# Three tiles of the leading expert worked out ahead of the full routing, instead of four

## The chip, the cores and the metric

The kernel runs on one core of a Trainium2 chip. The metric is the device time of one execution in microseconds (us). Engines are named as in the profile: PE is TensorE, ACT ScalarE, DVE VectorE, POOL GpSimd, SP SyncE.

## What is computed

Three layers in a row, on 4 sequences of 576 tokens with 512 channels (8 heads of 64):

```
q_s = softmax(q, axis=-1);  k_s = softmax(k, axis=2)
attn = q_s @ (k_s^T @ v)                                   # per head; 4 x 576 x 512
h = relu(x^T @ w_tok1) @ w_tok2;  u = x + h^T              # mixing over the tokens
x1 = u + relu(u @ w_ch1) @ w_ch2                           # 512 -> 1536 -> 512 channels
logits = x1 @ w_gate                                       # 8 experts
e[s] = argmax(logits[s]) where sigmoid(x1[s] @ w_local) < 0.5 or s == 0, else e[s-1]
out[s] = softmax(logits[s])[e[s]] * (relu(x1[s] @ w1[e]) @ w2[e])      # 512 -> 1024 -> 512
```

## The kernel before, in words

Every engine runs its own hand-ordered list of instructions; semaphores tie them together. What one engine waits for holds up all that stands behind it on that engine.

**Part one** works through the batches b = 0 to 3. The channel layer of a batch is 32 "chunks": per half of the tokens 12 chunks of the hidden layer (`hid`, 12 matmuls each) and 4 of its output (`y`, 36 matmuls each), numbered by `idx` 0 to 31. Products are kept nearly exact by splitting each operand into a rounded part (name with `_h`) and a rest (`_l`): ACT writes `hid_h`, DVE `hid_l`, for each chunk. PE may start chunk idx only when the outputs of chunk idx-2 are out (`chan_done`). Between the chunks of batch b stand the attention steps of batch b+1 for two groups of heads. The table `AT` (L304) says behind which chunk each step stands, on every engine that has a share in it, and the same table serves all three batches that have a next one. The steps spoken of below, all for group 0:

- `kmax` and `kmax2` (DVE, L1164): the maximum of the keys. `kmax` is one operation of 512 columns; `kmax2` is two of 256 columns into the tile shown as `lgp`. PE's step `mT` (`kmax_turn`, L517), behind chunk 5, transposes what `kmax2` leaves.
- `qT01` and `qT23` (PE, L547): ten transposes of the normalized queries. The first two need the first half of POOL's scaling (`pool_scale`, L1802, operation L1794), the next three the second half.

The weights of the channel layer are split once, at the start. ACT rounds them, and the rests `wc_l` of the 12 pieces of `w_ch2` are made by DVE for the even pieces (`split_second`) and by POOL for the odd ones (L1821), beside the first chunks.

**Part two** is the expert layer. Tokens of one expert are gathered into tiles of 128 rows. For a tile t PE does `hidden` (two halves of 12 matmuls, L783), transposes it (`h_turn`, L795), and does `output` (two halves of 12 matmuls, L808); `x_turn` (L725) transposes the gathered rows. DVE makes the rests `xgT_l` (`xgT_out`, before hidden half 0) and `hT_l` (`hT_out`, before output) and scales the result (`yo_out`). POOL gathers the rows of a tile and scatters its result with indirect DMAs.

Which token goes where is known only when the logits of all batches are. So a first routing of batches 0 to 2 (`route_early`) picks the expert with most tokens there, and its first `EARLY` tiles are run by straight-line code. Beside them DVE works out the full routing: `held_by_lanes`, `tiles_of_experts`, `rows_of_lanes`, `tiles_of_lanes`, `probabilities`, `values_of_lanes`, `row_lanes`. PE turns that into row numbers (`rows_of_tiles`, L826, 18 matmuls), DVE stores them (`ids_out`), POOL gathers tile number `EARLY`, and from there a loop over a table of tiles runs (`Fori`, L894) until all tiles are done. If the leading expert had fewer full tiles than `EARLY`, the missing ones would be run empty (`unfilled`). SP loads an expert's weights in 8 units of 512 KB; for the second expert it starts once the gathers of tiles `EARLY` and `EARLY + 1` have landed (L501 to L503), and ACT and DVE split the units inside the tiles.

## Time and profile before

| | us |
|---|---|
| median of 3 runs (728.61 to 729.15) | 728.89 |
| the profiled execution, its own time | 728.89 |
| its span in the profile | 726.8 |
| PE busy | 715.9 |
| DVE busy | 304.6 |
| ACT busy | 234.5 |
| POOL busy | 137.5 |

The 2.09 us between the span and the execution's own time lie outside what the profiler records. Times in the rows are microseconds from the start of the span. Part one runs until about 455, the early tiles until about 512, the loop of tiles from there.

### The profile page before, as it was taken

To read this page: it belongs to the slowest core of one execution; us is meant where nothing else is said; L and a number is where in the kernel's file an instruction comes from. 1 tells how busy PE (TensorE), PEld (TensorE's weight loads), DVE (VectorE), ACT (ScalarE), POOL (GpSimd) and SP (SyncE) were. 2 spreads that over 40 slices of the span, in tenths; PEclk is the share of its full clock that TensorE was granted. 3 is DMA by queue.
4 is the path that set the end of the run, shared out by engine and by line. 5 is a ranking of instruction groups with operands and counts; after the bars stand their busy time and mean duration, and the time that the engine had idled before them with its cause. 6 is when DMAs were issued, how large, how long until landed. Compare 5 with 4: busy or idle time off the path is not lost.

```text
span 726.8 us, 14345 instructions
## 1 busy us (share of the span) xinstructions
PE 715.9 (99%) x5016; PEld 650.9 (90%) x5017; DVE 304.6 (42%) x641; ACT 234.5 (32%) x452; POOL 137.5 (19%) x166
## 2 busy tenths in 40 slices
PE   7999999999999999999999999999999999999997
PEld 7799999999999999999999999788888888888885
DVE  5765332235332235332224822685445552221631
ACT  2773142023142023142021034321445542222621
POOL 5574020002020002020000016022221322121311
PEclk9999999999999999999999999999999999999999
DMA  9952131012131012100010340113744561010000
GB/s 224 376 108 67 33 99 33 1 35 67 33 99 33 1 35 67 33 33 1 1 38 2 116 163 16 54 44 125 289 159 139 180 238 58 23 52 29 34 22 12
DMA packets 71997, 57.65 MB, mean 79 GB/s; under 512 B 54892, under 2 KB 57228, under 8 KB 71952
## 3 DMA queue, kind: packets, MB, share of 16 engines
q1 hardware_dynamic: 68432, 47.58, 21.9%
q0 software_dynamic: 3520, 9.44, 3.9%
q8 instruction: 32, 0.52, 0.3%
q14 instruction: 13, 0.11, 0.0%
HBM read 48.79 MB, written 10.31 MB: 81 GB/s over the span
## 4 chain that ended last, share of the span: by engine, by line
PE 96%; DVE 2%; ACT 1%; issue 1%; POOL 0%; POOLq 0%; DVEq 0%
PE bank L640 42%; PE bank L783 16%; PE bank L808 15%; PE bank L572 5%; PE bank L603 3%; PE bank L795 2%; PE bank L595 2%; PE bank L671 2%; PE bank L725 1%; PE bank L515 1%; PE bank L543 1%; PE bank L560 1%; PE bank L582 1%; PE bank L648 1%; PE bank L529 0%
## 5 line engine op out<-in xcount | busy, mean ns | idle before, releaser
L640 PE MATMUL bank<-u_h,wc_h 128*128 128x288 f32 x384 | 117.2, 305 | 0.1
L640 PE MATMUL bank<-hid_h,wc_h 128*128 128x288 f32 x384 | 115.0, 300 | 0.0
L640 PE MATMUL bank<-hid_l,wc_h 128*128 128x288 f32 x384 | 113.2, 295 | 0.0
L640 PE MATMUL bank<-u_h,wc_l 128*128 128x288 f32 x384 | 113.1, 295 | 0.0
L640 PE MATMUL bank<-u_l,wc_h 128*128 128x288 f32 x384 | 113.1, 294 | 0.0
L640 PE MATMUL bank<-hid_h,wc_l 128*128 128x288 f32 x384 | 113.0, 294 | 0.0
L783 PE MATMUL bank<-wslots,xgT_h 128*128 (+1 forms) x344 | 110.6, 402 | 0.0
L808 PE MATMUL bank<-wslots,hT_h 128*128 (+1 forms) x336 | 104.2, 391 | 0.1
L1485 DVE SCALAR_TENSOR_TENSOR hid_l<-bank,hid_h 128x288 fp32r<-128x288 f32 x96 | 43.1, 454 | 108.7 <-ACT hid_h L989 108.2
L989 ACT ACTIVATE hid_h<-bank 128x288 fp32r<-128x288 f32 x96 | 39.3, 409 | 113.5 <-PE bank L640 113.1
L808 PEld LDWEIGHTS bank<-wslots,hT_h 128*128 128x128 f32 x336 | 62.6, 188 | 13.6 <-DVE hT_l L1691 0.7
L640 PEld LDWEIGHTS bank<-u_h,wc_h 128*128 128x128 f32 x384 | 72.1, 188 | 1.8 <-DVE hid_l L1485 1.0
L640 PEld LDWEIGHTS bank<-hid_h,wc_l 128*128 128x128 f32 x384 | 72.3, 188 | 0.0
L640 PEld LDWEIGHTS bank<-u_l,wc_h 128*128 128x128 f32 x384 | 72.2, 188 | 0.1
L640 PEld LDWEIGHTS bank<-hid_l,wc_h 128*128 128x128 f32 x384 | 72.2, 188 | 0.1
L640 PEld LDWEIGHTS bank<-hid_h,wc_h 128*128 128x128 f32 x384 | 72.0, 188 | 0.1
L640 PEld LDWEIGHTS bank<-u_h,wc_l 128*128 128x128 f32 x384 | 72.0, 188 | 0.0
L783 PEld LDWEIGHTS bank<-wslots,xgT_h 128*128 128x128 f32 x344 | 61.4, 189 | 11.3
L783 PE MATMUL bank<-wslots,xgT_l 128*128 (+1 forms) x172 | 67.8, 394 | 0.0
L808 PE MATMUL bank<-wslots,hT_l 128*128 (+1 forms) x168 | 65.6, 390 | 0.0
L1492 DVE TENSOR_TENSOR x1T<-bank,u_h 128x288 f32<-128x288 f32 x32 | 14.6, 457 | 115.7 <-PE bank L640 115.7
L1868 POOL DMA_INDIRECT out_dram<-yo,id_out x21 | 22.8, 1084 | 172.1 <-DVE yo L1702 172.1
(270 smaller groups left out, 1056.6 us busy)
## 6 DMA issues: line engine op xcount, KB each, us to landing
w1raw<-in_moe_w_dram SPq DMA_DIRECT2D x20, 512.0 KB, 5.3
w2raw<-in_moe_w_dram SPq DMA_DIRECT2D x20, 512.0 KB, 4.8
wc_raw<-in_moe_w_ch_dram SPq DMA_DIRECT2D x8, 768.0 KB, 10.3
vb<-in_v_dram SPq DMA_DIRECT2D x32, 128.0 KB, 3.2
x_rows<-x1n SPq DMA_DIRECT2D x16, 256.0 KB
kb<-in_k_dram SPq DMA_DIRECT2D x24, 128.0 KB, 2.9
qb<-in_q_dram SPq DMA_DIRECT2D x24, 128.0 KB, 2.9
qraw<-in_q_dram SPq DMA_DIRECT2D x2, 512.0 KB, 4.7
```

The costliest lines, as they stand in the source:

```text
L572: last = pe.matmul(mix_bank(n, g)[:, c * TOK:(c + 1) * TOK], queries(n)[:, i, c * P:(c + 1) * P], wt1[:, i, :], start=(i == 0), stop=(i == ...
L595: pe.matmul(bank[4 + j % 2][:, 0:HS], kvd[:, c // CG, c % CG, :], qT[:, c // CG, c % CG, part], start=True, stop=False)
L603: last = pe.matmul(bank[4 + j % 2][:, 0:HS], h1T[a][:, m, c * P:(c + 1) * P], wt2[x][:, m, part], start=False, stop=(m == KT - 1 and (a, x ...
L640: last = pe.matmul(to, lhsT, rhs, start=(m == 0), stop=(m == len(mms) - 1))
L671: last = pe.transpose(bank[7][0:size, c * P:(c + 1) * P], x1T[:, c, at:at + size], ident[:, :])
L783: last = pe.matmul(bank[half][:, :], xgT[a][:, c, :], w1s[x][:, bass.ds(n & 1, 1), c, half * 512:(half + 1) * 512].rearrange("p a n -> p ( ...
L795: last = pe.transpose(bank[2 + half][:, c * P:(c + 1) * P], hs[:, f * P:(f + 1) * P], ident[:, :])
L808: last = pe.matmul(bank[5][:, :], hT[a][:, f, :], w2s[x][:, bass.ds(n & 1, 1), f, :].rearrange("p a n -> p (a n)"), start=(f == 0 and (a, ...
L989: act.activation(hid[0][:, i, :], bank[idx % 2][:, 0:HS], ACT.Relu).then_inc(hid_hi, 1)
L1485: dve.scalar_tensor_tensor(out=hid[1][:, i, :], in0=psum, scalar=0.0, in1=hid[0][:, i, :], op0=ALU.max, op1=ALU.subtract).then_inc(chan_do ...
L1492: dve.tensor_tensor(x1T[:, i, :], psum, u[0][:, i, part], ALU.add).then_inc(y_sum, 1)
L1868: pool.indirect_dma_start(out=out.rearrange("b s d -> (b s) d"), out_offset=bass.IndirectOffsetOnAxis(ap=id_out[:, 0:1], axis=0), in_=yo[: ...
```

## The change

`EARLY` goes from 4 to 3. The straight-line code of tile 3 goes away on all engines and the loops begin at tile 3. PE's `rows_of_tiles` moves from behind the second `h_turn` of tile 2 to ahead of its first. On DVE `tiles_of_experts` and `rows_of_lanes` become one function, `slots_of_lanes`, and the pieces of the routing and the work for the tiles are interleaved in another order. On POOL the gathers of tiles 3 and 4 now stand ahead of the scatter of tile 1. In part one DVE makes the rests of pieces 0 to 4 of `w_ch2` and POOL those of 5 to 11, and three entries of the table `AT` change.

```diff
-    EARLY = 4
+    EARLY = 3
...
-        BY_VECTOR = (0, 2, 4, 6, 8, 10)
-        BY_POOL = (1, 3, 5, 7, 9, 11)
+        BY_VECTOR = 5
...
-            ("kmax", 0): 3, ("kmax2", 0): 3, ("mT", 0): 5, ("ksub", 0): 6, ("ksub2", 0): 6, ("kexp", 0): 6,
+            ("kmax", 0): 3, ("kmax2", 0): 4, ("mT", 0): 5, ("ksub", 0): 6, ("ksub2", 0): 6, ("kexp", 0): 6,
...
-            ("qrec2", 0): 7, ("kv", 0): 9, ("qT01", 0): 11, ("qT23", 0): 12, ("mix", 0): 12, ("h1", 0): 13,
+            ("qrec2", 0): 7, ("kv", 0): 9, ("qT01", 0): 10, ("qT23", 0): 11, ("mix", 0): 12, ("h1", 0): 13,
...
+            rows_of_tiles()
             h_turn(2, 0, True)
             hidden(2, 0, 1, True)
-            x_turn(3)
-            output(2, 0, 0, True)
+            output(2, 0, 0, True, FIRST)
             h_turn(2, 1, True)
-            rows_of_tiles()
...
-                if j in (3, 5, 7):
-                    split_second(j - 3)
+                if j >= 2 * KD - BY_VECTOR:
+                    split_second(j - (2 * KD - BY_VECTOR))
             for idx in range(HEAD):
                 chunk_out(0, idx)
-                split_second(2 * KD - 2 + 2 * idx)
...
+            probabilities(P, 2)
+            yo_out(0, False)
+
             hT_out(1, 0)
-            yo_out(0, False)
-
-            tiles_of_experts()
+            slots_of_lanes()
             xgT_out(2)
-            rows_of_lanes()
             tiles_of_lanes()
             hT_out(1, 1)
-            probabilities(P, 2)
             values_of_lanes()
+            row_lanes(P, rowhot, rows_hot)
             yo_out(1, True)
...
-            for c in BY_POOL:
+            for c in range(BY_VECTOR, KC):
...
             gather(2, EP * J)
             scatter(0, False)
-            pool.wait_ge(xgT_ready, 3)
-            gather(3, EP * J)
-            scatter(1, True)
...
             gather(EARLY, rows_in=xg3, id_of=id_in3, landed=x3_in)
-            pool.wait_ge(xgT_ready, EARLY)
+            pool.wait_ge(xgT_ready, 3)
             gather(EARLY + 1)
+            scatter(1, True)
```

Three places of the order of instructions. DVE beside chunks 3 and 4 of the first batch, before:

```order
L1485 SCALAR_TENSOR_TENSOR hid_l<-bank,hid_h 128x288
L1172 TENSOR_TENSOR kmax<-kb 128x512
L1175 TENSOR_TENSOR lgp<-kmax 128x256
L1178 TENSOR_TENSOR lgp<-lgp,kb 64x256
L1485 SCALAR_TENSOR_TENSOR hid_l<-bank,hid_h 128x288
L1214 TENSOR_REDUCE qmax<-qb 128x8
```

and with the change:

```order
L1470 SCALAR_TENSOR_TENSOR hid_l<-bank,hid_h 128x288
L1157 TENSOR_TENSOR kmax<-kb 128x512
L1470 SCALAR_TENSOR_TENSOR hid_l<-bank,hid_h 128x288
L1160 TENSOR_TENSOR lgp<-kmax 128x256
L1163 TENSOR_TENSOR lgp<-lgp,kb 64x256
L1199 TENSOR_REDUCE qmax<-qb 128x8
```

The two `lgp` operations (`kmax2`) now stand behind the `hid_l` of chunk 4, and so behind the end of that chunk on PE.

PE at the first ten transposes of the queries, before (the chunk behind them is the first `y` chunk):

```order
L640 MATMUL bank<-u_h,wc_h 128x288
L640 MATMUL bank<-u_l,wc_h 128x288
L640 MATMUL bank<-u_h,wc_l 128x288
L560 MATMUL bank<-ident,qb 128x128 x5
L640 MATMUL bank<-hid_h,wc_h 128x288
L640 MATMUL bank<-hid_l,wc_h 128x288
```

and with the change (behind them comes chunk 11 of the hidden layer):

```order
L639 MATMUL bank<-u_h,wc_h 128x288
L639 MATMUL bank<-u_l,wc_h 128x288
L639 MATMUL bank<-u_h,wc_l 128x288
L559 MATMUL bank<-ident,qb 128x128 x5
L639 MATMUL bank<-u_h,wc_h 128x288
L639 MATMUL bank<-u_l,wc_h 128x288
```

The five transposes of `qT01` moved one chunk of 12 matmuls ahead.

DVE in early tile 1, from the end of `held_by_lanes` (`held`, `own`) on, before:

```order
L1579 CAST held<-upto 128x8
L1344 TENSOR_TENSOR own<-chosen,code 128x144
L1691 TENSOR_TENSOR hT_l<-bank,hT_h 128x512
L1702 TENSOR_SCALAR yo<-bank,prob_t 128x512
L1584 TENSOR_TENSOR gt<-bank,step 128x144
```

and with the change (`den` to `prob_l` are `probabilities`):

```order
L1329 TENSOR_TENSOR own<-chosen,code 128x144
L1334 TENSOR_REDUCE den<-expl 128x18
L1335 TENSOR_TENSOR top<-expl,own 128x144
L1336 TENSOR_REDUCE prob<-top 128x18
L1337 TENSOR_SCALAR den<-den 128x18
L1338 RECIPROCAL den<-den 128x18
L1339 TENSOR_TENSOR prob<-prob,den 128x18
L1340 CAST prob_h<-prob 128x18
L1341 TENSOR_TENSOR prob_l<-prob,prob_h 128x18
L1684 TENSOR_SCALAR yo<-bank,prob_t 128x512
L1673 TENSOR_TENSOR hT_l<-bank,hT_h 128x512
L1568 TENSOR_TENSOR gt<-bank,step 128x144
```

The first `hT_l` of tile 1 moved behind the eight operations of `probabilities` and behind `yo` of tile 0; the operations of `slots_of_lanes` from `gt` on follow it, and the `xgT_l` of tile 2 stands behind all of them.

## Rows read from the trace of the kernel before

**Rows 1.** The page's busy times, and the longest of PE's four waits.

```profile
PE 715.9 (99%) x5016; PEld 650.9 (90%) x5017; DVE 304.6 (42%) x641; ACT 234.5 (32%) x452; POOL 137.5 (19%) x166
...
PE bank L515 <- POOL kvd L1783: 3.6, 1, 3.6
```

**Rows 2.** Timeline, batch 0: start, duration, engine, line, tiles, count; POOL, DVE, PE.

```profile
51.16 1.54 POOL L1823 TENSOR_TENSOR wc_l<-wc_raw,wc_h 128x512 fp32r<-128x512 f32 x1 [0.16 <-ACT wc_h L1044]
...
52.03 1.23 DVE L1172 TENSOR_TENSOR kmax<-kb 128x512 f32<-128x512 f32 x1
...
54.22 0.44 PE L522 MATMUL bank<-ident,lgp 128*128 128x128 f32 x2
```

**Rows 3.** Timeline, batch 1, the same step; DVE, ACT, PE.

```profile
161.43 0.68 DVE L1172 TENSOR_TENSOR kmax<-kb 128x512 f32<-128x512 f32 x1
162.14 0.42 DVE L1175 TENSOR_TENSOR lgp<-kmax 128x256 f32<-128x256 f32 x1
162.60 0.42 DVE L1178 TENSOR_TENSOR lgp<-lgp,kb 64x256 f32<-64x256 f32 x1
...
162.19 0.41 ACT L989 ACTIVATE hid_h<-bank 128x288 fp32r<-128x288 f32 x1 [1.17 <-PE bank L640]
...
163.57 0.38 PE L522 MATMUL bank<-ident,lgp 128*128 128x128 f32 x2
```

**Rows 4.** Timeline, batch 1, POOL's scaling; PE at chunk 10 and at `qT01`.

```profile
171.75 2.47 POOL L1794 TENSOR_TENSOR qb<-qb,qrec 128x512 f32<-128x512 f32 x2 [4.33 <-DVE qrec L1225]
...
172.03 0.40 PE L640 MATMUL bank<-u_h,wc_h 128*128 128x288 f32 x1
...
175.30 0.71 PE L560 MATMUL bank<-ident,qb 128*128 128x128 f32 x5
```

**Rows 5.** Timeline, early tiles 1 and 2, DVE.

```profile
473.42 0.31 DVE L1344 TENSOR_TENSOR own<-chosen,code 128x144 f32<-128x144 int32 x1
...
474.65 0.74 DVE L1702 TENSOR_SCALAR yo<-bank,prob_t 128x512 f32<-128x512 f32 x1
476.13 0.31 DVE L1584 TENSOR_TENSOR gt<-bank,step 128x144 f32<-128x144 f32 x1 [0.74 <-PE bank L824]
...
477.53 0.69 DVE L1476 TENSOR_TENSOR xgT_l<-bank,xgT_h 128x512 fp32r<-128x512 f32 x1
478.14 0.15 DVE L1593 SCALAR_TENSOR_TENSOR before_p<-first_tile,bank 128x8 f32<-128x8 f32 x1
...
480.41 0.68 DVE L1605 TENSOR_TENSOR tilehot<-sloti,lane 128x504 f32<-128x504 int32 x1
...
481.74 0.29 DVE L1349 TENSOR_REDUCE den<-expl 128x18 f32<-128x144 f32 x1
...
483.64 0.68 DVE L1361 TENSOR_TENSOR val<-tilehot,token 128x504 fp32r<-128x504 f32 x1
```

**Rows 6.** Timeline, early tiles 1 and 2, PE.

```profile
476.34 0.71 PE L808 MATMUL bank<-wslots,hT_h 128*128 128x512 f32 x2
...
479.52 0.71 PE L783 MATMUL bank<-wslots,xgT_h 128*128 128x512 f32 x2
...
491.85 2.18 PE L830 MATMUL bank<-val,rowhot 128*128 128x84 f32 x18
```

**Rows 7.** Timeline, gather of tile 4; issue to landing of all 23 gathers.

```profile
495.55 1.10 POOL L1856 DMA_INDIRECT xg<-x_rows,id_in  x1 [0.86 <-POOL id_in L1853]
...
DMA to landing us min/median/max: 2.1/3.5/6.0
```

**Rows 8.** POOL's DMA queue from 478 to 486: packets, MB, share.

```profile
q0 software_dynamic: 152, 0.49, 20.1%
```

**Rows 9.** First weight units of the second expert (502 to 506); ACT's first split.

```profile
L417 SPq DMA_DIRECT2D w1raw<-in_moe_w_dram x4: 333/338/351, 502.8 to 504.8; - x4
...
DMA to landing us min/median/max: 3.8/6.7/7.8
...
513.74 2.01 ACT L983 ACTIVATE wslots<-w1raw 128x1024 f32 x2 [0.44 <-issue]
```

More of the change, by code:

```diff
@@ L243, in build @@
             yo = sb(part2, "yo", [P, D])
-            sb(part2, "end_of_rows", [P, 1104])
+            sb(part2, "end_of_rows", [P, 1120])
             xg3 = sb(part2, "xg3", [P, D])
@@ L614, in second_ready @@
             def second_ready(f):
-                if f in BY_VECTOR:
-                    pe.wait_ge(wc2_lo, BY_VECTOR.index(f) + 1)
+                if f < BY_VECTOR:
+                    pe.wait_ge(wc2_lo, f + 1)
                 else:
-                    pe.wait_ge(wc2_lo_pool, BY_POOL.index(f) + 1)
+                    pe.wait_ge(wc2_lo_pool, f - BY_VECTOR + 1)
             def chunk(b, idx, first=False):
@@ L860, in _ @@
             output(1, 0, 1, True)
+            rows_of_tiles()
             h_turn(2, 0, True)
             hidden(2, 0, 1, True)
-            x_turn(3)
-            output(2, 0, 0, True)
+            output(2, 0, 0, True, FIRST)
             h_turn(2, 1, True)
-            rows_of_tiles()
-            hidden(3, 0, 0, True)
-            output(2, 0, 1, True)
-            h_turn(3, 0, True)
-            hidden(3, 0, 1, True)
-            output(3, 0, 0, True, FIRST)
-            h_turn(3, 1, True)
             x_turn(EARLY)
-            output(3, 0, 0, True, SECOND)
-            output(3, 0, 1, True, FIRST)
+            output(2, 0, 0, True, SECOND)
+            output(2, 0, 1, True, FIRST)
             pe.wait_ge(routed, 2)
             hidden(EARLY, version_of(EARLY), 0, True)
-            output(3, 0, 1, True, SECOND)
+            output(2, 0, 1, True, SECOND)
             def tile(t, again):
@@ L1127, in _ @@
             hs_out(2, 1)
-            xgT_out(3)
             hT_out(2, 1)
-            hs_out(3, 0)
-            hT_out(3, 0)
-            hs_out(3, 1)
-            hT_out(3, 1)
             xgT_out(EARLY)
@@ L1579, in held_by_lanes, with slots_of_lanes @@
                 then(dve.tensor_copy(held[:, :], upto[SCANS % 2][:, PAD + J - 1, :]), expert_chosen)
-            def tiles_of_experts():
+            def slots_of_lanes():
                 dve.wait_ge(ranks_ready, 1)
@@ L1589, in tiles_of_experts @@
                 then(dve.tensor_reduce(first_tile[:, :], ntb[:, :, :], AX_X, ALU.add))
-            def rows_of_lanes():
                 then(dve.scalar_tensor_tensor(out=before_p[:, :], in0=first_tile[:, 0:E], scalar=float(P), in1=bank[7][:, E:2 * E], op0=ALU.mult, op1=ALU.add))
@@ L1715, in _ @@
             own_expert(P)
+            probabilities(P, 2)
+            yo_out(0, False)
             hT_out(1, 0)
-            yo_out(0, False)
-            tiles_of_experts()
+            slots_of_lanes()
             xgT_out(2)
-            rows_of_lanes()
             tiles_of_lanes()
             hT_out(1, 1)
-            probabilities(P, 2)
             values_of_lanes()
+            row_lanes(P, rowhot, rows_hot)
             yo_out(1, True)
+            ids_out()
             hT_out(2, 0)
-            row_lanes(P, rowhot, rows_hot)
-            xgT_out(3)
-            hT_out(2, 1)
-            ids_out()
             versions()
             tables()
-            yo_out(2, True)
-            hT_out(3, 0)
+            hT_out(2, 1)
+            xgT_out(EARLY)
             plan_loads()
-            hT_out(3, 1)
-            xgT_out(EARLY)
             word = next_weights(EARLY - 1)
@@ L1904, in _ @@
             gather(EARLY, rows_in=xg3, id_of=id_in3, landed=x3_in)
-            pool.wait_ge(xgT_ready, EARLY)
+            pool.wait_ge(xgT_ready, 3)
             gather(EARLY + 1)
+            scatter(1, True)
             scatter(2, True)
-            scatter(3, True)
             pool.wait_ge(routed, 2)
```

## Prediction

> **What bounds the kernel now.** I read the page's busy times first, then PE's waits, then the timeline of all engines at the three places that the change touches. The page says that PE is busy 99% of the span, and the longest of its four waits, 3.6 us, is at the very start [rows 1]; from 60 us to the last tile the list of its waits is empty. So PE sets the time, and its work stays what it was: the same chunks, and the same tiles as long as the fourth early tile is not an empty one. It isn't. In the 8 us in which tile 3 is gathered and tile 0 scattered, POOL's DMA queue moved 0.49 MB [rows 8], and two full tiles of 128 rows of 2 KB are 0.52 MB. A tile taken out of the straight code comes back as one more turn of the loop. A gain could come only from a wait of PE that goes, and there is none to go; what can change is that new waits appear. Since PE has no slack later, each one stays in the time to the end. The sum is made against the profiled execution: 726.8 us of span and 728.89 in all, which is also the median, so what is added to the span is added to 728.89.
>
> **Part one: kmax2 behind chunk 4, three times.** Uncontended case, batch 1 [rows 3]. Before, DVE ran kmax at 161.43 and the pair kmax2 right behind it, done at 162.60 + 0.42 = 163.02. PE came to its transposes at 163.57, so the margin was 0.55. Now the hid_l of chunk 4 stands between. It can't start before ACT's hid_h is out, 162.19 + 0.41 = 162.60, and takes until about 163.01 (0.38 from its start to DVE's next, as between 477.53 and 478.14 for a longer one). The pair then runs 0.46 + 0.42 (from 162.14 to 162.60, and the second's 0.42) and is done at 163.89. PE waits until about 163.95 with a handover of 0.06: 0.38 us. The same holds in batch 2. That is **+0.76** for two batches.
>
> Batch 0 is another case, since POOL is splitting weights there. Kmax took 1.23 us in batch 0 and 0.68 in batch 1 [rows 2, 3]. It started at 52.03 while a POOL split ran from 51.16 to 52.70, and it ended 0.55 late, so it had waited for nearly all of the 0.67 that the POOL operation still had to go. In these rows a DVE operation with two operands in SBUF waits until POOL's running one is through, and the other way round (POOL's splits take 1.30 alone and up to 1.73 beside one on DVE).
>
> The Trainium skill ("SBUF — State Buffer", section "SBUF: two separate sides") says the same of the port pair that the two share: an exclusive lock for the whole instruction, the loser fully blocked. This rule speaks against the change, and the rows agree; without it the step below would cost as little as its lower bound, with it the upper one.
>
> With the change POOL has seven pieces in one run instead of six with gaps. Piece 5 can't start before 45.9 us (ACT has it ready then); at 1.30 each, with 0.35 for the DVE split beside piece 5, POOL is at piece 9 from 51.5 to 52.8, at piece 10 from 53.3 (after kmax) to 54.6, and at piece 11 behind it. DVE comes to the pair at 53.67. Its first operation waits for piece 10 and is done at about 54.9; piece 11 has the port by then, until about 56.15; the second is done at 56.45. PE goes on with chunk 6 at 56.65, instead of 54.58 = 54.22 and the 0.36 that its transposes and the wait behind them took [rows 2]: **+2.07**. The low end: if neither operation meets POOL, the pair is done at 53.67 + 0.88 = 54.55, PE goes on at 54.75, and the step costs 0.17; with one meeting, 0.9. I take 2.07, since kmax's row shows the meeting and POOL's run leaves no gap for the second.
>
> **qT01 behind chunk 10, three times.** The transposes of its second tile need POOL's second scaling. In batch 1 that ended at 171.75 + 2.47 = 174.22 [rows 4]. PE began chunk 10 at 172.03 and reached qT01 at 175.30, after 24 matmuls, so a chunk is 1.64. Now qT01 comes at 173.67, the first tile's two transposes go until 173.83, and the rest waits until 174.29: 0.46. POOL's scaling hangs on chunk 6 through DVE, ACT and DVE again, so the delay from kmax2 moves both ends and does not cover this. Batches 0 and 2 repeat it within 0.02. **+1.4** for three. The bounds: none if this chain gains half a microsecond, 0.6 each if it loses a little.
>
> **The splits themselves** cost nothing beside this. DVE loses one of six; the last rest is ready at about 56.5 instead of 52.7, and PE reads the first of them in the first y chunk, ten microseconds later (near 67).
>
> **Part two: DVE's new order in early tile 1.** DVE had finished `own` at 473.42 + 0.31 = 473.73. Now the eight operations of the probabilities come next; they took 483.64 - 481.74 = 1.90 [rows 5]. Behind them yo of tile 0 (0.70 to the next) and then hT_l of tile 1, at 476.35, done at 477.04. PE's output(1, half 0) stood at 476.34 [rows 6] and needs it: it starts at 477.1, **+0.75**. PE's whole queue stands behind this wait.
>
> Then slots_of_lanes: from gt to before_p's end of line it took (477.53 - 476.13) + (480.41 - 478.14) = 1.40 + 2.27 = 3.67 [rows 5]. Begun at 476.97, it lets the xgT_l of tile 2 start at 480.64 and finish at 481.33, where before it stood at 477.53 between its two parts. PE would come to hidden(2, half 0) 479.52 - 476.34 = 3.18 after the output, at 480.28; it waits until 481.38: **+1.1**. After these two PE is 1.85 late, and DVE is through: tilehot, hT_l, the values (1.9) and the three rowhot (2.7) end near 487.2. PE's rows_of_tiles comes at 486.95 and asks for the last third only 1.3 later. No wait there.
>
> The next is the gather of tile 3. Before, rows_of_tiles ran from 491.85 for about 2.0 and the gather was issued at 495.55 [rows 6, 7], 3.7 after its start. Now that gives 486.95 + 3.7 = 490.65, and the rows land 3.5 later, the median of all 23 gathers, at 494.15. PE gets to x_turn(3) after rows_of_tiles 2.0, a transpose 0.36, a hidden half 2.86, half an output half 1.37 and a transpose 0.36, at 493.9. **+0.25**; the quickest of the 23, 2.1, would make it nothing, the slowest, 6.0, would make it 2.7, and the median is what a queue without other traffic should be near. Behind it stand the tables (3.7 on DVE, done near 494.7, wanted at 497), and plan_loads (2.4, done near 498.8, wanted by ACT near 500). Both fit.
>
> **The weights of the second expert** come closer. SP's first unit went out at 502.8 and ACT's first split was at 513.74: 10.9 [rows 9]. The issue moves ahead by 495.55 - 490.65 = 4.9, the split by a whole tile of 12.3 less the 2.0 of delay. So 5.5 is left for the first unit, which lands in 3.8, and about 9.7 for the fourth, which went out 2.0 later and landed 7.8 after that, at 9.8. I cost it at nothing, since PE needs DVE's output there 0.4 late; up to 1.5 if the fourth unit holds up ACT in front of its share of the tile.
>
> **The sum.** 0.76 + 2.07 + 1.4 + 0.75 + 1.1 + 0.25 = 6.3. Time: 728.9 + 6.3 = **735.2 us**, 0.9% slower.
>
> **The rivals.** (1) *POOL and DVE hardly meet in batch 0*: the pair slips between two splits, and the step costs 0.17 to 0.9. For it: the moments are known only to some tenths. Against it: POOL's run has no gaps. Sum 4.4 to 5.2, time 733.3 to 734.1. (2) *The new order is absorbed*: the chains to kmaxT, qT01 and xgT_l run shorter than their rows, because queues on DVE and ACT fill differently, and only the 1.1 at xgT_l or less is left. Against it: each of the three waits was worked out from the same rows that show no margin. 728.9 to 730.3. (3) *Faster, an empty tile goes*: if the fourth early tile had carried no rows, one tile of 12.3 us would be saved, which decides over the 6.3 as soon as it is true: 722.9. Against it stand the 0.49 MB. A smaller way to the same side, PE's tail being shorter by one skipped turn of the loop, is worth a tenth at most. (4) *The weights come late*: the fourth unit lands after ACT wants it and the loop's first tile waits 1 to 1.5: 736.2 to 736.7.
>
> **How the numbers follow.** The sum as it stands has 0.55, rival 1 has 0.22, rival 4 has 0.10, rival 2 has 0.08, rival 3 and its like 0.05. The likeliest is the sum, 735.2. The range takes in the sum, rival 1, most of rival 4 and the low bounds of the qT01 term: 731.5 to 736.9. A measurement of this kernel can tell about 0.2% from no change, which is 1.5 us: slower by more than that 0.87, within it 0.08, faster 0.05.
>
> **What would show it.** Right: among PE's waits of the changed kernel one behind the transposes of lgp of about 2 in batch 0 and 0.4 in batches 1 and 2 (releaser DVE), three of 0.45 at the transposes of qb (releaser POOL), one at output of tile 1 of 0.75 (hT_l) and one at hidden of tile 2 of 1.1 (xgT_l); kmax2's operations in batch 0 longer than 0.42; the loop's tiles at 12.3 as before. Wrong: PE's list of waits as empty as before, or only 20 scatters. A second lgp operation of 0.42 in batch 0 would mean rival 1.

## The result, and the profile after the change

The changed kernel takes **733.87 us** (median of four runs, 733.62 to 734.16), against 728.99 for the kernel before in the same comparison (728.61 to 729.15). The ratio is 1.0067, with a 95% interval from 1.0050 to 1.0086: 4.9 us slower. The forecast was 735.2, with a range from 731.5 to 736.9. The profiled execution of the changed kernel has a span of 732.7 us and took 734.45 in all, so the two profiled executions are 5.9 apart on their spans.

Busy times (engine, us, share of the span, instructions) and PE's waits (line that waits, engine and tile waited for, us in total, times, longest):

```profile
PE 717.6 (98%) x5016; PEld 651.5 (89%) x5017; DVE 304.2 (42%) x640; ACT 234.6 (32%) x452; POOL 134.1 (18%) x167
...
PE bank L514 <- POOL kvd L1760: 3.6, 1, 3.6
PE bank L521 <- DVE lgp L1163: 2.1, 3, 1.7
PE bank L807 <- DVE hT_l L1673: 0.8, 1, 0.8
PE bank L782 <- DVE xgT_l L1461: 0.8, 1, 0.8
PE bank L559 <- DVE kvd L1187: 0.7, 1, 0.7
PE bank L724 <- DMA xg<-x_rows,id_in: 0.6, 1, 0.6
PE bank L559 <- POOL qb L1771: 0.5, 3, 0.2
```

PE executes the same 5016 matmuls as in [rows 1], so no tile went. What is new in the list of waits is what the prediction listed, in the same places and with the same releasers: three at the transposes of `lgp`, three at the transposes of `qb`, one at the output of tile 1, one at the hidden half of tile 2, one at the gathered rows of tile 3. The rows of 3.6 and of 0.7 (`kvd`; put down to `qb` in the kernel before), both ahead of 60 us, stood in the kernel before too.

The place of each loss is seen best by an *offset*: the start of a matmul in one trace less the start of the same matmul in the other. From before to after it is 0.61 at PE's first turn of the stream (11.4 us; ahead of everything that the change touches), 2.17 behind batch 0's `kmaxT`, 2.55 behind its `qT01`, then 2.97, 3.35, 3.76 and 4.15 behind the same two places of batches 1 and 2. It falls to 3.81 at 470 us (the section on the new part two alone tells why), and is 4.93 behind the output of tile 1, 6.01 at the hidden half of tile 2, 6.35 where the loop begins, and 6.35 in its last tile. So the change costs 6.35 - 0.61 = 5.74 us in PE's stream. The 0.61 belongs to that one execution: in the twelve traces of the experiments the same offset lies anywhere from -0.7 to 0.8, though none of them changes anything ahead of 11.4 us.

It is the moment at which TensorE's clock rises. From 3.62 us on PE runs 104 equal matmuls (L515) without a gap. This stretch (columns: stretch, its length, PE's busy time and count, granted clock, DMA share, GB/s) is of the kernel before:

```profile
8.00:9.00 1.00, 1.00 (x22) 1.00 1.43 219
```

and these of the changed kernel:

```profile
8.00:9.00 1.00, 1.00 (x12) 1.00 1.38 221
9.00:10.00 1.00, 1.00 (x21) 1.00 1.07 198
```

The same matmuls go at about 22 in a microsecond at the clock's upper level and about 12 at the lower one, and between 8 and 9 us the two traces stand on different sides of the rise. The clock column reads 1.00 all the same, because the trace holds no record of the clock ahead of 7.77 us before and 9.04 us after; from there on it records the full one. Half of the 1.27 between these two moments is 0.63. In the twelve other traces the first record lies between 6.30 and 9.43, and half of its distance from 7.77 is the offset at 11.4 us to within 0.1. So a comparison of the spans of single executions has an error of up to 1.5 us before anything else differs.

The way from 5.74 in PE's stream to 4.9 on the medians has two more parts, both behind PE's last matmul. From the last scatter's issue to the end of the span it takes 3.53 in all six traces with four early tiles and 3.11 or 3.12 in all eight with three: 0.42 less. And the part of an execution outside its span was 2.0 to 2.2 in the executions of the kernel before and 1.7 to 1.8 in those of all kernels with three early tiles (medians 2.09 and 1.73): 0.36 less. On the spans of the two profiled executions this makes 5.74 + 0.61 - 0.42 = 5.93, and on the time of an execution, without the moment of the clock, 5.74 - 0.42 - 0.36 = 4.96.

**Batch 0, the pair of kmax2.** DVE, POOL and PE on the timeline (start, us, engine, line, tiles):

```profile
52.62 1.08 DVE L1157 TENSOR_TENSOR kmax<-kb 128x512 f32<-128x512 f32 x1
53.82 0.46 DVE L1470 SCALAR_TENSOR_TENSOR hid_l<-bank,hid_h 128x288 fp32r<-128x288 f32 x1
54.20 0.93 DVE L1160 TENSOR_TENSOR lgp<-kmax 128x256 f32<-128x256 f32 x1
55.17 1.37 DVE L1163 TENSOR_TENSOR lgp<-lgp,kb 64x256 f32<-64x256 f32 x1
...
46.48 9.78 POOL L1800 TENSOR_TENSOR wc_l<-wc_raw,wc_h 128x512 fp32r<-128x512 f32 x7 [4.92 <-ACT wc_h L1035]
...
56.59 0.44 PE L521 MATMUL bank<-ident,lgp 128*128 128x128 f32 x2 [1.67 <-DVE lgp L1163]
```

POOL's seven pieces are one run without a gap, 46.48 to 56.26, 1.40 each. The two `lgp` operations, 0.42 each in an undisturbed batch [rows 3], take 0.93 and 1.37 beside it, and the second ends 0.28 behind the end of POOL's run. PE waits 1.67 for it.

**Batch 1**, the same two places:

```profile
165.56 0.41 DVE L1160 TENSOR_TENSOR lgp<-kmax 128x256 f32<-128x256 f32 x1
166.01 0.42 DVE L1163 TENSOR_TENSOR lgp<-lgp,kb 64x256 f32<-64x256 f32 x1
166.48 0.44 PE L521 MATMUL bank<-ident,lgp 128*128 128x128 f32 x2 [0.19 <-DVE lgp L1163]
...
176.69 0.38 PE L559 MATMUL bank<-ident,qb 128*128 128x128 f32 x2
177.24 0.55 PE L559 MATMUL bank<-ident,qb 128*128 128x128 f32 x3 [0.18 <-POOL qb L1771]
```

The waits read 0.19 and 0.18, yet the offset grows by 0.42 and 0.38. A row counts a wait from the modelled end of the matmul ahead, and in an undisturbed stream the next one starts well before that end: the last matmul ahead of the first wait began at 165.99 with 0.29 of duration, and the transposes at 166.48, which is 0.49 where two such matmuls follow each other by 0.13. For a small wait the offset is the price, not the row.

**Early tiles 1 and 2**, DVE, then PE:

```profile
477.58 0.31 DVE L1329 TENSOR_TENSOR own<-chosen,code 128x144 f32<-128x144 int32 x1
...
479.84 0.75 DVE L1684 TENSOR_SCALAR yo<-bank,prob_t 128x512 f32<-128x512 f32 x1
480.51 0.68 DVE L1673 TENSOR_TENSOR hT_l<-bank,hT_h 128x512 fp32r<-128x512 f32 x1
481.11 0.30 DVE L1568 TENSOR_TENSOR gt<-bank,step 128x144 f32<-128x144 f32 x1
...
484.79 0.69 DVE L1461 TENSOR_TENSOR xgT_l<-bank,xgT_h 128x512 fp32r<-128x512 f32 x1
...
481.25 0.73 PE L807 MATMUL bank<-wslots,hT_h 128*128 128x512 f32 x2 [0.85 <-DVE hT_l L1673]
...
485.53 0.73 PE L782 MATMUL bank<-wslots,xgT_h 128*128 128x512 f32 x2 [0.83 <-DVE xgT_l L1461]
```

From `own` to `hT_l` DVE now needs 2.93 (480.51 - 477.58), and from `gt` to `xgT_l` 3.68, where it was 1.40 before [rows 5]. PE waits for the result both times.

### The profile page after: what moved, and what is told of

Read it like the earlier page. It is cut to its first block, busy times and chain, and to the rows that moved or that the text cites. A ratio compares the mean times of both kernels' runs of the same rounds, so it can differ in the third digit from the quotient of the medians.

```text
span 732.7 us, 14448 instructions
## 1 busy us (share of the span) xinstructions
PE 717.6 (98%) x5016; PEld 651.5 (89%) x5017; DVE 304.2 (42%) x640; ACT 234.6 (32%) x452; POOL 134.1 (18%) x167
## 4 chain that ended last, share of the span: by engine, by line
PE 90%; DVE 4%; ACT 2%; POOL 1%; issue 1%; DMA 1%; POOLq 0%; DVEq 0%
PE bank L639 39%; PE bank L782 16%; PE bank L807 15%; PE bank L571 5%; PE bank L602 3%; PE bank L794 2%; PE bank L594 2%; PE bank L670 2%; PE bank L724 1%; PE bank L514 1%; POOL qb L1771 1%; PE bank L559 1%; PE bank L581 1%; PE bank L647 1%; DMA xg<-x_rows,id_in 1%
## 5 line engine op out<-in xcount | busy, mean ns | idle before, releaser
L1771 POOL TENSOR_TENSOR qb<-qb,qmax 128x512 f32<-128x512 f32 (+1 forms) x12 | 15.1, 1258 | 210.2 <-DVE qmax L1199 210.2
```

The costliest lines, as they stand in the source:

```text
L1771: pool.tensor_tensor(by_head(queries(n))[:, IHALF[part], :, :], x[:, IHALF[part], :, :], by[:, IHALF[part], :].unsqueeze(3).broadcast_to([ ...
```

## Experiments

Each kernel is one edit of the kernel before or of the changed kernel, run beside the kernel before on the same chip. All times are medians; the kernel before had 728.48 in the first set (`b_split`, `b_kmax2`, `b_qt`, `a_part2`), 728.75 in the second (`p2_hT_first`, `p2_order`, `p2_no_prob`), 728.51 in the third (`b_split_late`, `p2_both_first`, `p2_best`) and 728.36 in the last (`after_late`, `b_split_k2`). The single medians scatter by half a microsecond and more (in the five kernels of part one they lie from 0.3 below to 0.6 above what the offsets give), so the sizes of single steps are read from offsets of one trace each, and the ratios tell that nothing large is hidden elsewhere.

### The split of wc2 alone

```diff
-        BY_VECTOR = (0, 2, 4, 6, 8, 10)
-        BY_POOL = (1, 3, 5, 7, 9, 11)
+        BY_VECTOR = 5
...
-            for c in BY_POOL:
+            for c in range(BY_VECTOR, KC):
```

PE's waits for the rests and DVE's calls of `split_second` follow, as in the change.

> The kernel before with one edit: the rests of w_ch2's pieces 0 to 4 by DVE and 5 to 11 by POOL, as in the change; kmax2, qT01 and all of part two as before. Port theory (DVE's two-operand operations wait for POOL's running one): POOL is now in one run over chunks 3 to 5 of batch 0, so kmax2's two operations take about 0.9 and 1.4 us in place of 0.42 each although their place is the old one, hid_l of chunk 4 comes behind them, and PE begins chunk 6 about 1.9 late: 730.8. Rival (it was the place behind chunk 4 that cost, not the split): the two operations keep 0.42, no new wait of PE, 728.9.

Measured (`b_split`): 729.90, ratio 1.0019 [1.0009, 1.0029]. The offset jumps once, by 1.74 at chunk 6 of batch 0 (from 0.51 to 2.25), and is flat everywhere else in part one. DVE and PE there:

```profile
52.50 1.08 DVE L1171 TENSOR_TENSOR kmax<-kb 128x512 f32<-128x512 f32 x1
53.62 1.40 DVE L1174 TENSOR_TENSOR lgp<-kmax 128x256 f32<-128x256 f32 x1
55.05 1.37 DVE L1177 TENSOR_TENSOR lgp<-lgp,kb 64x256 f32<-64x256 f32 x1
...
56.47 0.44 PE L521 MATMUL bank<-ident,lgp 128*128 128x128 f32 x2 [1.67 <-DVE lgp L1177]
```

The pair stands where it stood before, directly behind `kmax`, and is late all the same: POOL's run alone makes both operations three times as long. The wait is the split's, not the place's. The cost was expected at 1.9; the offset has 1.74, and the median 1.4.

### The same split, POOL's last pieces elsewhere

```diff
-            for c in range(BY_VECTOR, KC):
-                pool.wait_ge(wc2_hi, c + 1)
-                pool.tensor_tensor(wc2[1][:, c, :], wc2_raw[:, c, :], wc2[0][:, c, :], ALU.subtract).then_inc(wc2_lo_pool, 1)
-            softmax_steps(NG)
+            pieces(5, 6, 7, 8)
+            pool_sub(NG)
+            pieces(9, 10, 11)
+            pool_scale(NG)
```

`pieces` holds the two lines of the old loop's body.

> b_split (kernel before with the change's split of w_ch2) with one edit on POOL: pieces 9 to 11 are made between the subtraction and the scaling of the next softmax instead of ahead of both. All pieces are made, only later; PE reads the first of them 10 us after. Port theory: at kmax and kmax2 of batch 0 POOL is idle, so kmax takes 0.68 and kmax2's operations 0.42 each, the 1.74 us that b_split lost come back, and the wait of 0.35 that the kernel before has at chunk 6 goes too: 728.1 to 728.5. Rival (DVE is slow there for its own five splits or for something else): the operations stay at about 0.9 and 1.4, 729.9.

Measured (`b_split_late`): 728.35, ratio 0.9995 [0.9986, 1.0004]; no wait for `lgp`.

```profile
46.68 5.40 POOL L1822 TENSOR_TENSOR wc_l<-wc_raw,wc_h 128x512 fp32r<-128x512 f32 x4 [4.92 <-ACT wc_h L1043]
...
52.81 0.68 DVE L1171 TENSOR_TENSOR kmax<-kb 128x512 f32<-128x512 f32 x1
53.53 0.42 DVE L1174 TENSOR_TENSOR lgp<-kmax 128x256 f32<-128x256 f32 x1
53.99 0.42 DVE L1177 TENSOR_TENSOR lgp<-lgp,kb 64x256 f32<-64x256 f32 x1
```

The same work on the same engine, only not at the same moment: with POOL's run ended at 52.08, `kmax` falls from 1.08 to 0.68 and the pair to 0.42 each. The whole 1.74 is gone, and 0.3 besides that the kernel before itself lost there (the offset goes from 0.79 to 0.48). In time that is not to be told from the kernel before. Together the two kernels show the cause. The Trainium skill ("SBUF — State Buffer", section "SBUF: two separate sides") has the rule, an exclusive lock between the two engines for a whole instruction; these rows agree with it, 0.42 against 0.93 to 1.40.

### kmax2 at chunk 4 alone

```diff
-            ("kmax", 0): 3, ("kmax2", 0): 3, ("mT", 0): 5,
+            ("kmax", 0): 3, ("kmax2", 0): 4, ("mT", 0): 5,
```

> The kernel before with one edit: kmax2 behind chunk 4 instead of 3. Port theory: in batch 0 POOL's pieces end at 52.7, before kmax2 starts, so its two operations keep 0.42 there and the step costs 0.1 to 0.2; in batches 1 and 2 PE waits about 0.4 each at the transposes of lgp, as in the changed kernel. Together about +1.0: 729.9. Rival (the place alone cost the 1.6 us of batch 0): +2.4, 731.3.

Measured (`b_kmax2`): 730.04, ratio 1.0018 [1.0008, 1.0028]. Offsets: 0.10 in batch 0, 0.41 and 0.40 in the other two.

```profile
PE bank L522 <- DVE lgp L1178: 0.6, 3, 0.2
```

The uncontended estimate of 0.38 for each of two batches was good. In batch 0 it is only 0.10: there the kernel before already lost 0.3 to `kmax` beside POOL's piece of 51.16 [rows 2], and the later place avoids that.

### Both together

Both diffs above, the first and the third.

> The kernel before with two parts of the change: the contiguous split of wc2 and kmax2 at chunk 4. By themselves they cost 1.74 and 0.92 (0.10 of it in batch 0). Theory (in batch 0 both hold the transposes to one event, the end of the second lgp, so that they overlap and do not add): the offset behind batch 0 is 1.5 to 1.7, plus 0.41 in each of the other two batches, 2.4 in all, 731.1 us. Rival (they add): 1.84 in batch 0 and 2.7 in all, 731.4. The last column of the difference is the wait for lgp in batch 0: 1.7 by the theory, 1.9 or more by the rival.

Measured (`b_split_k2`): 730.48, ratio 1.0029 [1.0018, 1.0039]. The offset grows by 1.56 in batch 0, 0.41 and 0.40 in the others, 2.36 in all.

```profile
PE bank L521 <- DVE lgp L1177: 2.1, 3, 1.7
```

The two parts don't add: 1.74 and 0.10 alone, 1.56 together. Both delay the same event, the end of the second `lgp` operation, and that is set by the end of POOL's run; started later, the first of the pair has less of a piece to wait for (0.93 instead of 1.40). 1.56 is to the hundredth what the changed kernel shows.

### qT01 and qT23 one chunk earlier, alone

```diff
-            ("qrec2", 0): 7, ("kv", 0): 9, ("qT01", 0): 11, ("qT23", 0): 12,
+            ("qrec2", 0): 7, ("kv", 0): 9, ("qT01", 0): 10, ("qT23", 0): 11,
```

> The kernel before with one edit: qT01 behind chunk 10 and qT23 behind 11. If the wait for POOL's second scaling is its own cost: three waits of PE at the transposes of qb, +0.38 each as between the two traces, +1.15 together: 730.1. If it is only a follow-up of the kmax2 delay: nothing, 728.9.

Measured (`b_qt`): 730.06, ratio 1.0020 [1.0011, 1.0030]. Offsets: 0.38, 0.40 and 0.40, 1.18 in all.

```profile
PE bank L560 <- POOL qb L1794: 0.5, 3, 0.2
```

### The changed kernel with POOL's last pieces elsewhere

The second diff of this section, in the changed kernel.

> The changed kernel whole, with one thing altered: POOL computes its last three pieces of wc2 (9, 10, 11) between the subtraction and the scaling of its softmax share, not ahead of both, as in b_split_late. Theory (in batch 0 the loss of 1.56 us is the locked port alone, and the earlier place of the transposes behind kmax2 costs there what it cost by itself, 0.1): kmax takes 0.68 and the two lgp 0.42 each, the wait of 1.7 for lgp in batch 0 is gone, the two waits of 0.2 in batches 1 and 2 stay; the offset at chunk 6 of batch 0 falls by about 1.5, a further 0.3 as in b_split_late, so some 732.1 us against 733.87 for the changed kernel. Rival (the wait in batch 0 has a part that the place alone makes once the split has moved): 0.4 stays at the transposes of batch 0, as in the other two batches, and the time is 732.4 to 732.6. In no case does it fall to that of the kernel before, since 3.5 us of batches 1 and 2, qT01 and the early tiles are untouched.

Measured (`after_late`): 732.67, ratio 1.0058 [1.0041, 1.0075]; 4.3 over the kernel before, where the changed kernel was 4.9 over it.

```profile
PE bank L521 <- DVE lgp L1163: 0.6, 3, 0.2
```

On the offsets this is the first theory: 1.48 of the 1.56 come back in batch 0, where the rival would have left 0.4 and the offset grows by 0.1, and what is left of the waits for `lgp` is 0.6 in three, as in the kernel with kmax2 alone. The further 0.3 that was expected did not come, since with kmax2 at chunk 4 the transposes have no margin to give. The medians show less of it, 0.6 us, and would fit the rival's number as well, with four runs from 731.98 to 732.96 and an interval of 2.5 us; they don't contradict 1.5, and don't show it.

### The new part two alone

The changed kernel with the three edits of part one undone.

> The changed kernel with part one as before (the split of w_ch2 and the three table entries put back): EARLY = 3 and the new order of part two alone. If the parts add up: no new wait before 450 us, the waits for hT_l of tile 1, xgT_l of tile 2 and the gather of tile 3 as in the changed kernel, +1.8 to 2.2: 730.7 to 731.1. If part two's waits came from the shift of part one: near 728.9.

Measured (`a_part2`): 730.28, ratio 1.0021 [1.0012, 1.0031].

Part one and part two don't touch each other: PE's waits here are those of the changed kernel in the early tiles, 0.8 for `hT_l` and 0.8 for `xgT_l`, and the offsets grow by 1.12 and 1.08 there. The wait for the gathered rows of tile 3 is missing.

Why 1.12, when the step in the prediction said 0.75? All traces but the one of before are 0.35 ahead of it from 470 us on. These two rows of DVE in the kernel before say why:

```profile
465.94 0.19 DVE L1314 SCALAR_TENSOR_TENSOR fresh<-lg,first 128x18 f32<-128x18 f32 x1 [0.91 <-issue]
...
469.11 0.69 DVE L1691 TENSOR_TENSOR hT_l<-bank,hT_h 128x512 fp32r<-128x512 f32 x1
```

The logits `lg` came late in that one execution, 3.24 us behind SP's issue at 462.70, where `a_part2` has 2.46 (462.80 to 465.26). So DVE's chain and the `hT_l` of tile 0 at its end ran late, and PE began its output at 469.85, right behind it. In the thirteen other traces the same way took 1.88 to 2.54, so the 3.24 is that execution's own. The pause of 0.35 stands in no row of PE's waits. Behind it DVE waits for PE (`cc`) in either case, so that DVE's later moments are the same, and what PE had gained it lost again at the wait for `hT_l`: 1.12 against a kernel before without that pause, 0.77 against the profiled one.

### The eight operations of the probabilities left out

In the kernel with the new part two. The kernel leaves out the probabilities of the rows routed in full; the two on-chip tensors that they fill, `prob_h` and `prob_l`, get other values once, ahead of this stretch. So the rows behind the early tiles are scaled wrongly.

```diff
+            then(dve.tensor_copy(prob_h[:, :], lane[:, 0:J]))
+            then(dve.tensor_copy(prob_l[:, :], lane[:, 0:J]))
...
             own_expert(P)
-            probabilities(P, 2)
             yo_out(0, False)
```

> a_part2 with the eight operations of the full routing's probabilities left out on DVE (the scale of the rows behind the early tiles is then not that of the reference); 1.9 us less work for DVE in that stretch. Theory (DVE's work is the limit): both waits go, rows_of_tiles finds its rowhot in time, what is left is the wait for the gather of tile 3, 0.3 or so: 729.2. Rival (the gather chain and not DVE is the limit): at least 1 us stays at x_turn(3), 730 or more.

Measured (`p2_no_prob`): 729.21, ratio 1.0006 [0.9996, 1.0015].

```profile
474.93 0.68 DVE L1675 TENSOR_TENSOR hT_l<-bank,hT_h 128x512 fp32r<-128x512 f32 x1
476.28 0.31 DVE L1570 TENSOR_TENSOR gt<-bank,step 128x144 f32<-128x144 f32 x1 [0.67 <-PE bank L824]
...
479.97 0.69 DVE L1462 TENSOR_TENSOR xgT_l<-bank,xgT_h 128x512 fp32r<-128x512 f32 x1
...
480.71 0.73 PE L783 MATMUL bank<-wslots,xgT_h 128*128 128x512 f32 x2 [0.80 <-DVE xgT_l L1462]
```

The wait at the output is gone, so the 1.90 of the probabilities made it. The wait at the hidden half is not gone, although 1.9 of work on DVE is. DVE now stands idle for 0.67 ahead of `gt`, since `gt` reads ranks that PE delivers with `before_b` ([rows 5] show the same kind of wait, 0.74); from there to `xgT_l` it is 3.7 by whatever way DVE comes to it. The sum of DVE's work was not the limit at that place. The time is the 729.2 that was expected, but not for the reason given: one of the two waits stayed, and in this trace the offset grows by 1.1 from 476 us to the last tile. The chain is PE's ranks, then `slots_of_lanes` whole, then `xgT_l`. Its cause is that `slots_of_lanes` was joined ahead of `xgT_out(2)`: in the last two kernels of this section its second part stands behind `xgT_out(2)`, and the wait is gone.

### hT_l of tile 1 ahead of the probabilities

```diff
             own_expert(P)
+            hT_out(1, 0)
             probabilities(P, 2)
             yo_out(0, False)
 
-            hT_out(1, 0)
             slots_of_lanes()
```

> a_part2 (EARLY = 3, part one as before) with one edit: on DVE hT_out(1, 0) stands ahead of the probabilities and of yo_out(0). If the two waits are costs of their own, as my sum has them: the wait for hT_l goes, 0.75 saved. Rival (DVE works without a gap there, and only the moment at which it comes to xgT_l of tile 2 counts): the wait for hT_l goes and the wait for xgT_l grows from about 1 to about 1.9, the time stays that of a_part2.

Measured (`p2_hT_first`): 729.51, ratio 1.0015 [1.0006, 1.0025]. DVE, then PE:

```profile
473.07 0.69 DVE L1675 TENSOR_TENSOR hT_l<-bank,hT_h 128x512 fp32r<-128x512 f32 x1
...
475.58 0.75 DVE L1686 TENSOR_SCALAR yo<-bank,prob_t 128x512 f32<-128x512 f32 x1
...
476.43 0.70 PE L808 MATMUL bank<-wslots,hT_h 128*128 128x512 f32 x2 [0.89 <-issue]
```

Both expectations missed the waits: the one at the output stayed, and the one at `xgT_l` did not grow (0.8). Only the rival's time held: from 476 us to the last tile the offset grows by 1.9, as in `a_part2`; the two medians, from different sets, lie 0.8 apart. `hT_l` is ready at 473.76, and PE still starts its output at 476.43, 0.1 behind the end of `yo`. The output of tile 1 writes the bank that `yo` of tile 0 reads, so PE waits for both. The row doesn't name a releaser ("issue"), and in the changed kernel the row names only the later one. The prediction's step was right in size because the two operations are neighbours there.

### Both ahead of the probabilities

```diff
-            probabilities(P, 2)
-            yo_out(0, False)
-
             hT_out(1, 0)
+            yo_out(0, False)
+            probabilities(P, 2)
             slots_of_lanes()
```

> a_part2 with hT_out(1, 0) and yo_out(0) ahead of the probabilities on DVE (p2_hT_first moved hT alone, and PE's output also needs yo of the tile before to be out of bank 5). If DVE works without a gap from there to xgT_l of tile 2: the wait at output goes and the wait at xgT_l grows from 1.1 to about 2.1, time as a_part2. If the two waits are costs of their own: 1.1 saved, 729.2.

Measured (`p2_both_first`): 730.96, ratio 1.0030 [1.0018, 1.0042]. The wait at the output is gone, the other has grown to 1.9, as it must where the probabilities are in front of `gt`. But the kernel is not equal to the one with the new part two; in the traces it is 1.5 later behind this place, on the medians 0.7 (six runs, 729.41 to 731.90). The rest is in the stretch behind the wait (columns: stretch, its length, busy time and count of PE, PEld, DVE, ACT, POOL, granted clock, DMA share, GB/s):

```profile
481.23 0.73 PE L783 MATMUL bank<-wslots,xgT_h 128*128 128x512 f32 x2 [1.93 <-DVE xgT_l L1462]
...
476.00:482.00 6.00, 4.07 (x21) 3.19 (x20) 5.38 (x21) 1.35 (x3) 0.96 (x1) 1.00 0.11 44
482.00:485.40 3.40, 3.40 (x9) 2.61 (x8) 3.37 (x6) 0.00 (x0) 0.00 (x0) 0.51 0.00 0
```

For 3.4 us the granted clock is 0.51, the lower of the two levels, 1.2 GHz. The hidden half takes 4.44 instead of 2.85, so 1.6 is added to a wait of 1.9.

### DVE's order of before in the new part two

```diff
-            probabilities(P, 2)
-            yo_out(0, False)
-
             hT_out(1, 0)
-            slots_of_lanes()
+            yo_out(0, False)
+            tiles_of_experts()
             xgT_out(2)
+            rows_of_lanes()
             tiles_of_lanes()
             hT_out(1, 1)
+            probabilities(P, 2)
             values_of_lanes()
```

> a_part2 with DVE's pieces in the order of the kernel before (hT_l and yo first, xgT_l of tile 2 between the tile counts and the slots, the probabilities behind hT_l of half 1), only the three rowhot ahead of yo of tile 1. Order theory (the new order of DVE costs): the waits for hT_l and xgT_l go and PE gains nearly all of part two back, 729.2. Rival (DVE's total work up to the last rowhot is the limit, since rows_of_tiles now stands ahead of tile 2's transposes): both waits go and one of 1.5 to 1.8 at rows_of_tiles takes their place; the time stays within 0.3 of a_part2.

Measured (`p2_order`): 730.91, ratio 1.0034 [1.0023, 1.0046]; 0.7 later in the traces than with the new order, 0.6 on the medians.

```profile
PE bank L830 <- DVE rowhot L1352: 1.3, 1, 1.3
PE bank L725 <- DMA xg<-x_rows,id_in: 1.1, 1, 1.1
```

Both waits of the early tiles go, and two others take their place. The rival had named the first of them, at 1.5 to 1.8, and not the second, at the gathered rows; its "within 0.3" was missed. With three early tiles instead of four `rows_of_tiles` stands one hidden and one output earlier in PE's stream, and DVE can't have the rows ready by then. So the new order is no mistake beside `EARLY = 3`: it is where the same work was put so that the larger waits don't arise, and from 476 us to the last tile the offset grows by 1.93 with it and by 2.67 with the old one.

### An order between the two

```diff
+            hT_out(1, 0)
+            yo_out(0, False)
             probabilities(P, 2)
-            yo_out(0, False)
-
-            hT_out(1, 0)
-            slots_of_lanes()
+            tiles_of_experts()
             xgT_out(2)
-            tiles_of_lanes()
+            rows_of_lanes()
             hT_out(1, 1)
+            tiles_of_lanes()
             values_of_lanes()
```

> EARLY = 3 with the order on DVE that I work out as the best for it: hT_l, yo, probabilities, tile counts, xgT_l of tile 2, slots, hT_l of half 1, tilehot, values, rowhot. No wait at output and none at xgT_l; but DVE's third rowhot is out only at about 487.5, and PE asks for it from 486.4 on, so about 1.0 is lost there and about 0.3 at the gather: 0.7 better than a_part2, still about 1.2 over the kernel before. Rival (only the order cost, three tiles hide the routing as well as four): the time of the kernel before.

Measured (`p2_best`): 729.60, ratio 1.0015 [1.0005, 1.0024].

```profile
PE bank L830 <- DVE rowhot L1352: 0.5, 1, 0.5
...
487.50:491.20 3.70, 3.70 (x14) 3.09 (x14) 2.30 (x10) 0.60 (x1) 1.51 (x3) 0.54 0.15 19
```

Only one wait of 0.5 is left in that stretch, and yet the trace is 0.4 later than with the new order: behind `rows_of_tiles` the granted clock was 0.54 for 3.7 us, which cost 1.35 in that hidden half. The median is 0.7 better than that of the new order alone, as expected, but the trace shows neither the 1.0 at the rows nor the 0.3 at the gather that made up the expectation; 0.7 is within what such medians scatter, so the number was met by luck. No order tried brought the three early tiles to the time of the kernel before, where PE has no wait in that stretch at all.

## Why the prediction was right

**What bounds the kernel** held in the main. PE's work is unchanged, it had no slack, and the new waits stayed: the offset is 6.35 in the loop's first tile and in its last. But "there is none to go" went too far. The kernel before had two short pauses of PE that the list of waits doesn't show. One is the 0.35 of the late logits. The other stands in early tile 3, at a weight load of PE (`PEld`), on the timeline of before:

```profile
506.45 0.30 PEld L808 LDWEIGHTS bank<-wslots,hT_h 128*128 128x128 f32 x2 [0.47 <-DVE hT_l L1691]
```

`b_kmax2` and `b_qt` have this pause too. `b_split` has none at this place, and its offset falls there by 0.38 (1.92 to 1.54). In the changed kernel that tile is one of the loop, and PE has no pause there either.

**Part one, kmax2 in batches 1 and 2**: forecast 0.76, measured 0.42 and 0.41 in the changed kernel, 0.83. **Batch 0**: forecast 2.07, measured 1.56. The mechanism is the one named, and `b_split` and `b_split_late` show it by putting it on and taking it off. The size was off by the end of POOL's run: the step counted 1.30 for a piece and added the collisions by hand, which put the end of the last piece at 56.15; it was at 55.65 in before's time (56.26 less 0.61), 1.40 a piece with all collisions. The wait for the first of the pair was shorter for the same reason. Rival 1, that the two hardly meet, fell with the second `lgp` operation of 1.37.

**qT01**: forecast 1.4 for three, measured 0.38, 0.38 and 0.39, and 1.18 by itself. In batch 1 of `b_qt` POOL's scaling ends at 175.33 and the third transpose begins 0.05 behind it, as forecast; PE comes to `qT01` at 174.83, which is 173.73 in before's time (it is 1.10 late there), and not 173.67. That is most of the 0.08 by which the term was too large each time.

**Part two**: forecast 0.75 and 1.1, measured 0.77 against the profiled execution (1.12 without its late logits) and 1.08. The prediction put `rows_of_tiles` at 486.95 in before's time; it stands at 491.10, less the 4.16 that it was late already, 486.94. The reasons were not complete, though. At the output the step named `hT_l`, and `yo` holds PE just as long (`p2_hT_first`). At the hidden half it counted DVE's time from the end of the first chain, but the start of `gt` is also bound by the ranks, and without the probabilities the wait stays at 0.80 (`p2_no_prob`).

**The gather of tile 3**: forecast 0.25; the wait is there, 0.55 in its row. PE comes to it at 494.09 in before's time (forecast 493.9), and the rows are in 4.1 after the issue instead of 3.5. The term was too small by more than its row says. In `a_part2`, which has the same instructions in part two, the rows are in time, 3.4 behind their issue or sooner; the changed kernel is 3.85 behind that trace ahead of `x_turn(3)` and 4.50 behind it from there on. So the wait cost 0.65. From the hidden half of tile 2 to the loop the offset against the kernel before grows by only 0.34, since the pause of 0.38 of early tile 3 goes in the same stretch; 0.65 - 0.38 leaves 0.07 unaccounted for. In `after_late` the gather costs 0.1, but PE pauses between 510 and 514 for another 0.5, so that its stretch grows by a like amount, 0.3, for other reasons. Why this gather took 4.1, and that of `a_part2` no more than 3.4, no run tells.

**The weights of the second expert**: forecast nothing, and right. SP issues the first unit at 501.80 and ACT's first split begins at 507.50, 5.7 later (forecast 5.5); PE has no wait behind it. Rival 4 fell. So did rival 3, with the 5016 matmuls and 21 scatters, and rival 2, with the list of waits.

**The sum**: 1.56 + 0.83 + 1.15 + 0.77 + 1.08 + 0.34 = 5.73, against 5.74 by the offset and 6.3 forecast; 0.5 of the excess is kmax2 in batch 0 and 0.25 is qT01. The prediction added what goes into PE's stream to the whole time, and had only "a tenth at most" for a shorter tail. The tail gave back 0.42 in the span and 0.36 outside it. The 0.42 is one turn of the loop, on POOL and not on PE: the number of turns that the loop is built for has `EARLY` in it (`NT`, L65), and behind the last scatter POOL steps through the unused ones, 0.44 each by its register and branch instructions in the trace (the views leave them out), six with four early tiles and five with three. Why the 0.36 goes is open. 5.74 - 0.78 = 4.96, beside 4.88 on the medians. If the kernel before is taken without its late logits, it is 5.3, and the medians can't tell the two apart. That 4.9 lies nearer to rival 1's 4.4 to 5.2 than to the sum's 6.3 is not for rival 1's reason: the pair met POOL's run in full. By the ratios the parts add up: 0.0029 (`b_split_k2`), 0.0020 (`b_qt`) and 0.0021 (`a_part2`) make 0.0070, and the whole has 0.0067.

## What to carry to other kernels

Where one engine has no wait left, an operation that another engine runs earlier or later costs what it goes beyond the margin that its reader had, and that can be worked out from the timeline of the kernel before (here to 0.1 us at seven of the nine new waits, and to 0.5 at the worst); the order of instructions has to be worked through to the last operand, buffers to be freed among them. Two engines that lock each other out, as DVE and POOL do here, should not be given back-to-back streams at the same time: here a run of seven pieces cost 1.7 us only because of when it ran, and nothing once its last three pieces stood two operations later. One profile against one profile has an error of its own, here of up to 1.5 us from the first microseconds alone; starts of the same instruction, less their offset at a place that nothing has changed yet, are free of it. Where an early start is taken away (one early tile less), look for what it had covered: no reordering tried here gave that cover back.

## What the runs showed of the hardware

A wait of PE can cost more than its own length. In `p2_both_first` a wait of 1.93 (in the six us to 482.00, the wait in them, PE was busy 4.07) was followed by 3.4 us at a granted clock of 0.51, and these cost a further 1.6. In `p2_best` a wait of 0.5 and eighteen narrow matmuls (128x84) were followed by 3.7 us at 0.54, which cost 1.35. Waits of nearly the same size elsewhere kept the full clock, by these stretches of the changed kernel around its two waits:

```profile
479.70:482.00 2.30, 1.45 (x10) 1.12 (x10) 2.16 (x7) 1.14 (x2) 0.47 (x1) 1.00 0.00 0
482.00:486.00 4.00, 3.17 (x16) 2.43 (x16) 3.65 (x13) 0.60 (x1) 0.56 (x1) 1.00 0.16 66
```

The wait of 1.67 in batch 0 and the ones of 1.3 and 1.1 in `p2_order` kept it too, although the same eighteen narrow matmuls follow the 1.3 there. So neither the length of the wait nor the narrow matmuls by themselves settle it; what does is open. Of two orders with nearly the same sum of waits the one with two small ones was the faster here: the new part two by itself, with 0.84 and 0.82, is 1.5 us ahead of the single wait of 1.93. Each of the two clock drops was seen in one profiled execution, and how often they come no run tells: on the medians `p2_both_first` is only 0.7 behind `a_part2`.
